# Routing rounds of 47 units and another order of loads, stores and VectorE work in a kernel of attention, a dense layer and eight experts

## What is computed

```python
def _attn_ref(q, k, v):                      # 4 x 8 heads x 768 x 64
    for t in range(S):
        state = gamma * state + k[:, :, t] (x) v[:, :, t]
        y[:, :, t] = scale * q[:, :, t] @ state

def _moe_ref(x, w_in, w_out, s, b):          # 3072 tokens, 512 -> 2048 -> 512
    r = np.maximum(x @ w_in, 0.0)
    return (s * (r * r) + b) @ w_out

def _moe2_ref(x, w_gate, w1, w2):            # 8 experts, 512 -> 1024 -> 512
    cap = N // E                             # 384 tokens each
    order = np.argsort(-(x @ w_gate).flatten())
    for idx in order:                        # best free pair of token and expert first
        tok, e = idx // E, idx % E
        if assigned[tok] >= 0 or counts[e] >= cap: continue
        assigned[tok] = e; counts[e] += 1
    for e in range(E):
        out[mask_e] = np.maximum(x[mask_e] @ w1[e], 0.0) @ w2[e]
```

## Time and profile before

| | us |
|---|---|
| median of three runs | 984.82 |
| lowest, highest | 984.60, 986.34 |
| the profiled execution | 984.82 |
| its span in the profile | 983.0 |
| TensorE's matmuls, busy | 967.5 |
| VectorE, busy | 515.4 |
| ScalarE, busy | 292.6 |
| GpSimd, busy | 214.0 |

### The profile page before, as it was taken

The page is one execution under the profiler, slowest core; times in us unless marked ns, Lnnn a source line. Parts: engine busy times, 40 slices in busy tenths (PEclk is TensorE's granted clock), DMA queues, the critical chain, the costliest instruction groups (busy, mean ns, idle before and its releaser), DMA issues.

```text
span 983.0 us, 15671 instructions
## 1 busy us (share of the span) xinstructions
PE 967.5 (98%) x6132; PEld 789.3 (80%) x6132; DVE 515.4 (52%) x1097; ACT 292.6 (30%) x527; POOL 214.0 (22%) x190
## 2 busy tenths in 40 slices
PE   7999999999999999999999999999999999999997
PEld 6777877878787777777777777777899998998996
DVE  4656555555555546556676666663344244244420
ACT  2443433334343445101010101010335354443521
POOL 4202111220112000000111111100326435534611
PEclk9999999999999999999999999999999999999999
DMA  9966555565555456957575757456635456546500
GB/s 312 359 206 248 203 212 215 201 220 209 211 214 197 161 197 231 343 178 231 196 234 191 233 186 230 156 159 192 214 112 193 130 160 204 161 135 198 172 33 33
DMA packets 80537, 193.29 MB, mean 197 GB/s; under 512 B 9680, under 2 KB 18128, under 8 KB 79952
## 3 DMA queue, kind: packets, MB, share of 16 engines
q1 hardware_dynamic: 76624, 179.71, 53.8%
q0 software_dynamic: 3840, 12.59, 3.9%
HBM read 129.08 MB, written 63.18 MB: 196 GB/s over the span
## 4 chain that ended last, share of the span: by engine, by line
PE 93%; DMA 3%; DVE 1%; SPq 1%; issue 1%; ACT 0%; POOLq 0%; POOL 0%; DVEq 0%
PE bank L901 26%; PE bank L1007 26%; PE bank L1048 14%; PE bank L1063 13%; PE bank L855 2%; PE bank L780 2%; PE bank L818 2%; DMA staging<-in_w_in 2%; PE bank L811 2%; PE bank L933 1%; PE bank L795 1%; PE bank L1028 1%; DMA early_qT<-in_q_turned 1%; DMA g_late<-g_rows 1%; PE bank L958 0%
## 5 line engine op out<-in xcount | busy, mean ns | idle before, releaser
L901 PE MATMUL bank<-x,wi_hi 128*128 128x512 f32 x768 | 240.9, 395 | 2.3 <-issue 1.6
L901 PEld LDWEIGHTS bank<-x,wi_hi 128*128 128x128 f32 x768 | 141.5, 188 | 51.1 <-issue 17.8
L620 POOL TENSOR_TENSOR w_lo<-w_raw,w_hi 128x512 fp32r<-128x512 f32 x72 | 93.6, 1308 | 299.7 <-ACT w_hi L729 299.5
L901 PE MATMUL bank<-x,wi_lo 128*128 128x512 f32 x384 | 149.8, 390 | 0.0
L1118 DVE SCALAR_TENSOR_TENSOR u_sb<-u_sb,sc_s 128x512 f32<-128x512 f32 x96 | 74.0, 770 | 132.2 <-ACT u_sb L661 132.1
L1007 PE MATMUL bank<-wo_b,g_back 128*128 128x512 f32 x552 | 138.0, 400 | 0.0
L729 ACT ACTIVATE w_hi<-w_raw 128x512 fp32r<-128x512 f32 x128 | 76.7, 636 | 164.7 <-DMA w_raw<-in_w 164.3
L661 ACT ACTIVATE u_sb<-bank 128x512 f32<-128x512 f32 x96 | 57.3, 597 | 201.2 <-PE bank L901 192.6
L1007 PEld LDWEIGHTS bank<-wo_b,g_back 128*128 128x128 f32 x552 | 99.4, 189 | 18.9 <-issue 0.8
L1389 DVE TENSOR_TENSOR w_lo<-w_raw,w_hi 128x512 fp32r<-128x512 f32 x56 | 59.8, 1067 | 67.6 <-ACT w_hi L729 66.9
L1048 PE MATMUL bank<-xg_hi,w_hi 128*128 128x384 f32 x256 | 86.9, 339 | 0.0
(11 more groups left out here) (184 smaller groups left out, 1238.6 us busy)
## 6 DMA issues: line engine op xcount, KB each, us to landing
g_rows<-g_sb SPq DMA_DIRECT2D x96, 512.0 KB, 2.9
g_back<-g_rows SPq DMA_DIRECT2D x80, 512.0 KB, 3.9
w_raw<-in_w SPq DMA_DIRECT2D x128, 256.0 KB, 3.8
x_rows<-x SPq DMA_DIRECT2D x24, 256.0 KB, 4.7
g_back<-g_rows SPq DMA_DIRECT2D x16, 384.0 KB, 4.4
kT<-in_k_turned SPq DMA_DIRECT2D x22, 256.0 KB, 3.6
qT<-in_q_turned SPq DMA_DIRECT2D x22, 256.0 KB, 3.6
vin<-in_v SPq DMA_DIRECT2D x22, 256.0 KB, 4.3
```

Source lines behind the costliest of these rows:

```text
L620: pool.tensor_tensor(low, w_raw[:, (p * E_PIECES + n) % RAW, :], high.bitcast(F32), ALU.subtract).then_inc(w1_lo_done, 1)
L901: last = pe.matmul(up[i % 2][:, :], w[:, t, fs], x[:, half, t, :], start=(t == 0 and n_ == 0), stop=(t == DT - 1 and n_ == 2))
```

## The change

Four edits. A round of the routing has 47 units instead of 48 (round r comes r units earlier), and the eighth expert's rank stands 5 units behind the seventh's instead of 6. On VectorE places(), the spreads and where() each move one pass ahead, to passes 0, 1, 2 and 3. The first two turnings stand one unit earlier. On SP, the four row tiles of a block are stored together at the ninth step of the next block instead of one at each of four steps (in the last block that is step 88 instead of 84 to 87), the loads of g_late are issued at the last block's steps 84 to 95, four more behind them, all ahead of the stores of tiles 20 to 22, and the second expert's number and its first six weight loads stand ahead of the wait for the gathers and the store of tile 23.

```diff
-LATE_TURN_AT = {len(DOWN_UNITS) - 4: 0, len(DOWN_UNITS) - 2: 1}
+LATE_TURN_AT = {len(DOWN_UNITS) - 5: 0, len(DOWN_UNITS) - 3: 1}
...
-ROUND_AT, ROUND = 11, 48
+ROUND_AT, ROUND = 11, 47
...
-ROUTE[_at + RANK_AT + 6] = ("rank", EXPERTS - 1, 0)
+ROUTE[_at + RANK_AT + 5] = ("rank", EXPERTS - 1, 0)
...
-                blk, f = divmod(i, FT)
-                first_store = LOADS if blk < N_BLK - 1 else LOADS // 2
-                if blk and first_store <= f < first_store + CPB:
-                    store_row((blk - 1) * CPB + f - first_store)
-                if blk == N_BLK - 1 and f >= LOADS:
-                    load_late(f - LOADS)
+                if i % FT == LOADS and i > FT:
+                    for tile in range((i // FT - 1) * CPB, i // FT * CPB):
+                        store_row(tile)
+                if i >= STEPS - FT + LOADS // 2:
+                    load_late(i - (STEPS - FT + LOADS // 2))
+            for f in range(FT - LOADS // 2, FT):
+                load_late(f)
             for tile in range(TILES - CPB, LATE):
                 store_row(tile)
-            for f in range(FT - LOADS, FT):
-                load_late(f)
+            second = expert_number(1)
+            for n in range(RAW):
+                load_weights(1, n, second)
             for j in range(CT):
                 sp.wait_ge(gathered[j], 16)
             store_row(LATE)
-            second = expert_number(1)
-            for n in range(E_PIECES):
+            for n in range(RAW, E_PIECES):
                 load_weights(1, n, second)
...
                     if r:
-                        if k_ == 1:
+                        if k_ == 0:
                             places()
-                        elif k_ in (2, 3):
-                            spread(k_ - 2)
-                        elif k_ == 4:
+                        elif k_ in (1, 2):
+                            spread(k_ - 1)
+                        elif k_ == 3:
                             where()
```

## The result

The changed kernel takes **990.28 us** (median of five runs, 988.64 to 992.2) against 984.82 us for the kernel before on the same chip: a ratio of 1.0054 (95% interval 1.0037 to 1.007), 5.5 us slower. The forecast was 987.5 us, with a range up to 989.8. The profiled run took 991.07 us with a span of 989.2.

The account below looks back on a forecast made before the run. TensorE was taken to bound the kernel, carrying 93% of the chain of waits in a 983.0 us span. The terms -0.8+0.75+0.75+0.8+0.4+0.8 = +2.7 us on 984.8 gave 987.5 us, range 983.0 to 989.8.

Parts of the forecast that it names:

- late votes: Routing: VectorE's spreads one pass earlier end two late votes that TensorE waits for, -0.8 us (bounds -0.5 and -1.0).
- vote 0 of round 4: Routing: GpSimd's subtraction, at 547.83 before, stretches VectorE's chain, now without spare time, so TensorE waits, +0.75 us.
- hit in round 5: Routing: GpSimd's subtraction, at 618.42 before, falls 1.7 us behind the rank's start and holds up VectorE, +0.75 us.
- rank 7: Eighth expert's rank: VectorE finishes late by 0.1 us already, by 0.8 with a GpSimd subtraction, +0.8 us.
- g_back in the last block: Step 89: four stores at once, 1 MB, delay its load, +0.4 us (bounds -0.1 and +1.5).
- tail, the wait: Tile 23: g_late's 2.1 us loss goes, but a 6.3 us gather delays the third turning to 697.6, +0.8 us.
- From its landing G the rest is fixed: Tile 23: from the first gather's landing, G, turnings and units take 5.5 us, then the third turning starts.
- The hits: Routing: three GpSimd subtractions stretch VectorE operations that TensorE waits for, 2.3 us together (bounds 0.1 and 3.3).
- Rival 1: Tail: the gather only shares with the weight loads, takes 4.6 us; tail -0.9 instead of +0.8, 985.8 us; chance 0.19.
- Rival 2: Routing, rank to vote 0, rounds 3 to 6: subtractions cost 0.1 us, not 2.3; 985.3 us; chance 0.14.
- Rival 3: Last block: the stores delay loads 89 to 92, costing 1.5 to 3 us; 988.6 to 990.1 us; chance 0.10.

Follow-up runs that it names:

- busy_at_gather: Changed kernel with six more 128x512 matmuls, product thrown away, on TensorE ahead of its wait for gather 0; 989.07 us, ratio 1.0035.
- stall_short: late_loads_only with TensorE made to wait once, six steps before the first product's end, for one GpSimd fill of a dead buffer; 985.82 us, ratio 0.9998.
- second block: Second set of four experiments on one chip, with the changed kernel once more at 991.06 us beside the kernel before at 985.93 us.
- weights_back: Changed kernel with the second expert's first six weight loads back behind the gathers' wait and tile 23's store; 985.24 us, ratio 0.9989.
- queue_alone: Kernel before with the change's SP order and earlier turnings, rounds of 48 units; 989.94 us, ratio 1.0038.
- changed_again: Changed kernel unchanged, run once more beside the kernel before; 991.06 us, ratio 1.0058.
- routing_alone: Kernel before with the routing edits alone (rounds of 47, eighth rank 5 units behind, VectorE work one pass earlier); 988.46 us, ratio 1.0027.
- stores_back: Changed kernel with the row stores one per step again, in the last block at steps 84 to 87; 991.68 us, ratio 1.0063.
- combined: Kernel before with earlier g_late loads, VectorE's new order, and GpSimd's eleventh first-expert subtraction held until rank_done stood at 6; 988.41 us, ratio 1.0031.
- stall_long: late_loads_only with TensorE made to wait once, six steps before the first product's end, for three GpSimd fills of a dead buffer; 989.76 us, ratio 1.0030.
- turnings_back: Changed kernel with the first two turnings one unit later again, as before the change; 987.94 us, ratio 1.0028.
- late_loads_only: Kernel before with the earlier loads of g_late alone; 984.20 us, ratio 0.9979, and 983.82 us, ratio 0.9979, when run again.
- later_sub: Kernel before with earlier g_late loads, VectorE's new order, and GpSimd's eighth first-expert subtraction held until round 4's second vote; 984.23 us, ratio 0.9982.

## Why the prediction was wrong in size and right in sign

Each term beside what the trace of the changed kernel shows for it:

| term of the sum | predicted | in the profile |
|---|---|---|
| late votes | -0.8 | -0.8 |
| vote 0 of round 4 | +0.75 | +0.85 |
| hit in round 5 | +0.75 | 0.0 |
| rank 7 | +0.8 | +0.54 |
| g_back in the last block | +0.4 | +1.4 |
| tail, the wait | +0.8 | +0.75 |
| tail, half clock behind it | none | +1.6 |
| ahead of the routing | none | +1.8 |
| sum | +2.7 | +6.1 |

**The step that failed** is in the tail: "From its landing G the rest is fixed: ... 5.5". The wait itself was sized well: 6.3 us predicted for the gather, 6.4 measured, and a wait of TensorE "2 to 3 us", measured 2.77. But what follows on a wait of that length is not fixed. 6.93 us went from first to third turning instead of the 5.32 that busy_at_gather shows. I priced TensorE's wait at its length, and in this kernel it costs 1.6 us more. In every profile with a wait of TensorE of 2.7 us or more in the second product or the stall (2.77, 2.79, 2.94, 3.06, 3.18, 3.73) the clock fell within a microsecond of its end; of six waits between 1.1 and 2.5 us there (1.16, 1.36, 1.37, 1.70, 1.88, 2.49) one was followed by it, that of 1.88. With this term the forecast would have been 989.1 us, 1.2 short of the 990.28 measured. Behind a wait of TensorE of 2.58 us or more the clock fell near 10 us of the span too, in all four profiles that have one there, while one of 2.50 was not followed by it; a wait of 1.83 near 47 us in stall_short was. So in these eighteen profiles each wait of 2.58 us or more was followed by it, and shorter ones sometimes were; the length of the wait alone doesn't decide it.

That the other terms add up to the +2.7 predicted for them (-0.8+0.85+0.54+1.4+0.75) is luck: the hit in round 5 did not come, rank 7 cost less, and g_back cost 1.0 more than its term.

**Ahead of the routing** nothing was predicted and nothing belongs to the change. The 1.8 us are the stretch at 61.4 us (about 1.6) and 0.2 of scatter at the start. The error here was to take the one profiled run of before, with its clock of 0.999 for the whole, as the kernel's usual course: in the later blocks its medians were 985.8 to 986.4 us. So 1 to 1.5 of the 6.2 us by which the two profiles differ are the luck of the first profile. The medians, 5.5 us apart in the first set and 5.1 in the second block (991.06 and 985.93), share little of that luck, and the change's own terms in the table sum to 4.3. The other 0.8 to 1.2 us I can't assign.

**g_back.** The mechanism was right (SyncE issues the four stores from 660.81 to 663.80, so the load for step 89 goes out at 664.87 and lands 5.6 us later, 1.4 too late), and 1.4 was within its bounds. It isn't the same in each run: 1.36, 0.85, 0.67 and under 0.3 us in the profiles of changed, weights_back, queue_alone and changed_again. With 0.4 I was near the middle of these. In the other four kernels with the burst of stores the wait was under 0.3 as well.

**The hits** were right as a mechanism and counted as if the places of the subtractions were known to half a microsecond. They aren't: the one of round 5 stood at R+1.7 in my reckoning and at R-0.4 in the changed kernel (618.31 and 618.72), so it cost nothing; in routing_alone and stores_back it stood at R+0.4 and hit. The one at rank 7 met only an operation near its end and cost 0.54. On which operations it can hold, the rule of the Trainium skill ("SBUF — State Buffer", section "SBUF: two separate sides") agrees with the trace as far as it goes: the stretched ones (L1233 with 1.41 us, L1299 and L1300 with 1.15 and 1.19) end with a subtraction that started ahead of them, or within 0.2 us of it, and L1233 and L1300 have several inputs in SBUF. L1299 has one; by the rule it would have to be in a two-port mode, which no row here shows. That operations which read PSUM run through, as the prediction took from the rule, is borne out by combined: 0.19 and 0.20 us for L1294 and L1295 beside a subtraction.

**Rival 1**, that the gather only shares, fell by the six loads (6.1 us and more) and stood by the two (3.5 us). The rule of the Trainium skill ("DMA: Bandwidth & Descriptors", section "Queues, rings and completion order") is that each DMA engine goes round between the rings it has work for, packet by packet. Read as the prediction read it, it would let a gather with six loads in flight land about as soon as beside the late loads, where routing_alone has 4.2 us. The measured 6.1 to 7.4 us decide against that reading as a means of sizing; whether the engines go round so is not shown either way.

**Rival 2**, that VectorE's chain has room, is refuted for round 4: without the hit the ranks stand 36.41 us apart instead of 37.26. For round 5 of the changed kernel, where the subtraction missed, it held. **Rival 3**, 1.5 us or more at g_back, did not come about, and stores_back shows that the stores are not what made the kernel slow.

## What to carry to other kernels

Price a new wait of TensorE of some microseconds not only at its length but at the slower work behind it as well, here 1.6 us. And look at the granted clock right behind each wait in the windows, since no list of waits shows it. A transfer moved earlier "to use a free queue" is not free if a short transfer on which an engine waits is issued among its pieces; here six loads that nobody needed early cost 5 to 6 us, the wait and the half clock behind it together, and two of them cost nothing. Before an order is changed to win tenths in a chain that another engine disturbs, look at where that engine's operations fall, and compare two profiles of the same kernel to know what a difference between profiles is worth.

## What was not expected of the hardware

- TensorE's granted clock stood at 0.50 for 3.4 us behind every wait of TensorE of 2.58 us or more, in four different places (near 10 us of the span, the first product in stall_long, the owner's count of round 5 in combined, the first turning). It cost 1.6 us at the turnings (6.93 against 5.32 us) and 1.8 at the stall (5.0 us for a wait of 3.18). Of the waits between 1.8 and 2.5 us, two (1.83 and 1.88) were followed by it and others, up to 2.50, were not.
- The same stretch of 3.4 us comes near 60 us in most profiles, without a wait of a microsecond just ahead, and was absent in four of eighteen (before, turnings_back, late_loads_only, later_sub), with the same code up to there. It begins during or up to 1.1 us behind a row of 32 matmuls of 8 columns. Its cause is open.
- The gather of 128 rows took 3.5 us with two loads of 256 KB issued 1 to 2 us ahead of it and 6.1 to 7.4 us with six issued around it (from 1.8 us ahead to 1 us behind).
